# A kernel with a chunked linear recurrence: score matmuls per head over 64 rows, and the upper three levels' scores copied by ScalarE

## What is computed

```python
for t in range(S):
    cur = einsum('bhd,bhe->bhde', u * k[t], v[t])
    y[t] = einsum('bhd,bhde->bhe', r[t], state + cur)
    state = w[t][..., None] * state + einsum('bhd,bhe->bhde', k[t], v[t])
x = x + relu(norm(x) @ w_ch1) @ w_ch2
u_, v_ = split(relu(x @ w_in)); out = (u_ * (w_spatial @ norm(v_) + b)) @ w_out
```

## Time and profile before

| | |
|---|---|
| runs, median | 484.99 us (484.53 to 485.33) |
| profiled execution, span | 483.2 us, first to last instruction |
| TensorE busy | 438.5 us |
| VectorE busy | 282.0 us |
| ScalarE busy | 209.3 us |
| GpSimd busy | 150.2 us |

### The profile page before, as it was taken

The page is one execution under the profiler, slowest core; times in us unless marked ns, Lnnn a source line. Parts: engine busy times, 40 slices in busy tenths (PEclk is TensorE's granted clock), DMA queues, the critical chain, the costliest instruction groups (busy, mean ns, idle before and its releaser), DMA issues.

```text
span 483.2 us, 7994 instructions
## 1 busy us (share of the span) xinstructions
PE 438.5 (91%) x2724; PEld 413.5 (86%) x2724; DVE 282.0 (58%) x600; ACT 209.3 (43%) x486; POOL 150.2 (31%) x234
## 2 busy tenths in 40 slices
PE   3688779877877799999999999999999999999997
PEld 3587669776767689999999999999999998898997
DVE  6999999999999997124422432333241684413120
ACT  4787667667776673322212321332221752211211
POOL 6586666668776673600000000100010530000000
PEclk9999997799999999999999999999999999999999
DMA  7434432334432112200000000000410110010102
GB/s 222 139 79 118 116 99 72 85 92 123 124 85 72 50 36 68 65 1 0 1 0 1 1 1 1 0 1 0 152 44 1 33 34 2 0 50 1 50 1 97
DMA packets 26540, 25.59 MB, mean 53 GB/s; under 512 B 1666, under 2 KB 21890, under 8 KB 26500
## 3 DMA queue, kind: packets, MB, share of 16 engines
q1 hardware_dynamic: 26500, 25.08, 17.7%
HBM read 22.72 MB, written 2.36 MB: 52 GB/s over the span
## 4 chain that ended last, share of the span: by engine, by line
PE 63%; DVE 7%; issue 2%; ACT 1%; POOL 0%; DVEq 0%; ACTq 0%
PE bank L1122 20%; PE bank L1124 19%; PE bank L1123 19%; DVE score L773 3%; DVE wtot L731 2%; PE bank L1100 1%; PE bank L1207 1%; PE bank L1028 1%; DVE rin L750 1%; DVE sdec L804 1%; DVE ku L783 0%; PE bank L1069 0%; PE bank L1071 0%; PE bank L1070 0%; DVE state L820 0%
## 5 line engine op out<-in xcount | busy, mean ns | idle before, releaser
L1028 PE MATMUL bank<-rz,k 128*128 128x128 f32 x576 | 85.4, 295 | 28.9 <-DVE score L773 15.2
L1028 PEld LDWEIGHTS bank<-rz,k 128*128 128x128 f32 x576 | 74.3, 202 | 38.0 <-issue 36.7
L572 ACT COPY rz<-rin 64x256 f32<-64x256 f32 x144 | 58.7, 408 | 42.7 <-DVE rin L750 36.6
L773 DVE COPY_PREDICATED score<-msk,bank 128x512 f32<-128x512 int32 x84 | 74.0, 881 | 0.9
L511 POOL TENSOR_TENSOR vrstd<-vmv,half 128x1 f32<-128x1 f32 x12 | 7.7, 643 | 156.5 <-DVE vmv L974 156.5
L494 POOL TENSOR_TENSOR k<-k,wtot 128x256 f32<-128x256 f32 x60 | 42.8, 714 | 1.6
L466 POOL TENSOR_TENSOR k<-kin,ucol 128x128 f32<-128x128 f32 (+2 forms) x72 | 22.4, 311 | 54.5 <-ACT k L597 53.3
L887 DVE SCALAR_TENSOR_TENSOR h11l<-bank,h11h 128x384 fp32r<-128x384 f32 x24 | 13.4, 557 | 37.4 <-ACT h11h L660 37.4
L750 DVE TENSOR_TENSOR rin<-rin,wtot 128x256 f32<-128x256 f32 x60 | 32.8, 547 | 3.0 <-ACT rz L572 2.7
L660 ACT ACTIVATE h10h<-bank 128x384 fp32r<-128x384 f32 x24 | 11.8, 490 | 51.2 <-PE bank L1124 51.2
L887 DVE SCALAR_TENSOR_TENSOR h10l<-bank,h10h 128x384 fp32r<-128x384 f32 x24 | 13.4, 557 | 34.4 <-ACT h10h L660 34.4
(11 more groups left out here) (158 smaller groups left out, 1162.7 us busy)
## 6 DMA issues: line engine op xcount, KB each, us to landing
stage<-in_w SPq DMA_DIRECT2D x12, 384.0 KB, 3.3
vin<-in_v SPq DMA_DIRECT2D x12, 288.0 KB, 2.8
rin<-in_rT SPq DMA_DIRECT2D x12, 256.0 KB, 4.4
win<-in_wT SPq DMA_DIRECT2D x12, 256.0 KB, 3.6
kin<-in_kT SPq DMA_DIRECT2D x12, 256.0 KB, 4.4
out<-ob SPq DMA_DIRECT2D x12, 192.0 KB, 1.9
stage<-in_w_in SPq DMA_DIRECT2D x4, 384.0 KB, 3.2
x<-in_w_sp SPq DMA_DIRECT2D x4, 384.0 KB, 5.0
```

Source lines behind the costliest of these rows:

```text
L572: last = sc.copy(dst, src[lo:hi, :, :, :])
L773: ve.copy_predicated(dst, mb, src).then_inc(scores_placed, 1)
L1028: mm = te.matmul(b_level[n % 3][:, a * P:(a + 1) * P], kk[:, a, :], rz[l][:, a, :, :].rearrange("p e t -> p (e t)"), start=True, stop=True)
```

## The change

Two edits are made together. First, the padded `rz[l]` becomes `rc[l]`, the right half of r without padding, one copy of 128 partitions in place of two of 64. `level` issues eight matmuls where it issued four: each reads 64 partitions (one head) and 64 columns, the two heads of a pair write different banks of `b_level[n % 2]`, two pairs of banks in place of three banks. `b_y` has one bank in place of two. Second, levels 4, 5 and 6 (c = 16, 32, 64) are no longer selected by VectorE: ScalarE copies their whole blocks out of PSUM (`place_blocks`): 4, 2 and 1 copies. Since a block copy leaves the diagonal out, `with_u` runs for levels 0 to 3 alone, and the own term covers tokens 0, 16, 32 and so on (N_OWN = 8 of a tile) instead of token 0 alone, placed under a mask. The memsets of the padding go away.

```diff
@@ -309,6 +314,14 @@
             return sum(carries(j) and not first(j) for j in range(i + 1))
 
         HALF = [(0, 64), (64, 128)]
+
+        def level_taken(eng, n):
+
+            i, l = n // NL, n % NL
+            if l < N_MASKED:
+                eng.wait_ge(scores_placed, N_MASKED * i + l + 1)
+            else:
+                eng.wait_ge(blocks_placed, N_BLOCK * i + l - N_MASKED + 1)
 
         def split_waits(eng, n):
 
@@ -550,7 +562,7 @@
         def _(act):
             sc = nc.scalar
 
-            def pad(i, l):
+            def take_right(i, l):
 
                 q = i % 2
                 if l == 0:
@@ -561,18 +573,10 @@
                     src = halves(rin[i % 4][:, :, :], LEVELS[l])[1]
                 if i > 0:
                     act.wait_ge(level_done, NL * (i - 1) + l + 1)
-                elif l % 2 == 0:
-                    act.wait_ge(zeroed_by_pool, l // 2 + 1)
-                else:
-                    act.wait_ge(zeroed_by_vector, l // 2 + 1)
-                for e, (lo, hi) in enumerate(HALF):
-                    dst = rz[l][lo:hi, :, e, :]
-                    if l:
-                        dst = dst.rearrange("p a (m c) -> p a m c", c=LEVELS[l])
-                        last = sc.copy(dst, src[lo:hi, :, :, :])
-                    else:
-                        last = sc.copy(dst, src[lo:hi, :, :])
-                last.then_inc(padded_r_ready if l else padded_r0_ready, 1)
+                dst = rc[l][:, :, :]
+                if l:
+                    dst = dst.rearrange("p a (m c) -> p a m c", c=LEVELS[l])
+                sc.copy(dst, src).then_inc(right_r_ready if l else right_r0_ready, 1)
 
             def k_pairs(i):
 
@@ -616,6 +620,19 @@
                 if part != 0:
                     op.then_inc(weight_hi_ready, 1)
 
+            def place_blocks(i, l):
+
+                n, c = NL * i + l, LEVELS[l]
+                act.wait_ge(level_done, n + 1)
+                act.wait_ge(scores_placed, N_MASKED * (i + 1))
+                act.wait_ge(own_in_score, i + 1)
+                src = b_level[n % 2][:, :, 0:BANK // 2].rearrange("p e (a t) -> p e a t", a=NPR)
+                for m in range(P // (2 * c)):
+                    s0 = 2 * c * m
+                    last = sc.copy(score[i % 2][s0:s0 + c, :, :, s0 + c:s0 + 2 * c],
+                                   src[s0:s0 + c, :, :, m * c:(m + 1) * c])
+                last.then_inc(blocks_placed, 1)
+
             def take_kt(i):
                 act.wait_ge(k_turned, carried(i))
                 if i >= 2:
@@ -624,21 +641,21 @@
 
             def take_x(i):
                 act.wait_ge(y_done, i + 1)
-                sc.copy(x[:, i, :], b_y[i % 2][:, 0:D]).then_inc(x_ready, 1)
+                sc.copy(x[:, i, :], b_y[:, 0:D]).then_inc(x_ready, 1)
 
             def split_vn(i):
                 b, c = i // CH, i % CH
                 act.wait_ge(vn_ready, i + 1)
                 sc.copy(vns[b][0][:, c * DH:(c + 1) * DH], vn[:, i, :]).then_inc(vn_hi_ready, 1)
 
-            pad(0, 0)
+            take_right(0, 0)
             k_pairs(0)
             k_right(0, 0)
             for i in range(NT):
                 for l in range(1, NL):
-                    pad(i, l)
+                    take_right(i, l)
                     if l == 5 and i + 1 < NT:
-                        pad(i + 1, 0)
+                        take_right(i + 1, 0)
                     k_right(i, l)
                     if l == 2 and i >= 1 and carries(i - 1):
                         take_kt(i - 1)
@@ -754,22 +776,20 @@
 
                 q = i % 2
                 dve.wait_ge(level_done, NL * i + l + 1)
-                if NL * i + l > 0:
-                    dve.wait_ge(scores_placed, NL * i + l)
+                if i + l > 0:
+                    dve.wait_ge(scores_placed, N_MASKED * i + l)
                 if l == 0 and i >= 2:
                     dve.wait_ge(y_done, i - 1)
-                src = b_level[(NL * i + l) % 3][:, :].rearrange("p (h t) -> p h t", h=H)
-                mk = msk[:, l, :]
+                src = b_level[(NL * i + l) % 2][:, :, 0:BANK // 2].rearrange("p e (a t) -> p e a t", a=NPR)
+                heads = score[q][:, :, :, :].rearrange("p e a t -> p (e a) t")
+                mk = msk[:, l * P // 2:(l + 1) * P // 2]
                 if l == 0:
-                    dst = score[q][:, :, :].rearrange("p h (m two) -> p h m two", two=2)[:, :, :, 1]
+                    dst = heads.rearrange("p h (m two) -> p h m two", two=2)[:, :, :, 1]
                     mb = mk[:, None, :].to_broadcast([P, H, P // 2])
                 else:
                     c = LEVELS[l]
-                    dst = halves(score[q][:, :, :], c)[1]
-                    src = src.rearrange("p h (m c) -> p h m c", c=c)
+                    dst = halves(heads, c)[1]
                     mb = mk.rearrange("p (m c) -> p m c", c=c)[:, None, :, :].to_broadcast([P, H, P // (2 * c), c])
-                if l == NL - 1:
-                    dst, src, mb = dst[:, :, 0, :], src[:, :, 0, :], mb[:, :, 0, :]
                 ve.copy_predicated(dst, mb, src).then_inc(scores_placed, 1)
 
             def own_product(i):
@@ -780,21 +800,23 @@
                     dve.wait_ge(own_parts_set, 3)
                 if i >= 1:
                     dve.wait_ge(own_ruk_ready, 2 * i)
-                ve.tensor_tensor(ku0[:, :, :], kin[i % 3][:, :, 0:1], ucol[:, :, None], ALU.mult).then_inc(
-                    own_uk_ready, 1)
+                ve.tensor_tensor(ku0[:, :, :], kin[i % 3][:, :, 0:P:STEP], ucol[:, :, None].to_broadcast([P, NPR, N_OWN]),
+                                 ALU.mult).then_inc(own_uk_ready, 1)
                 dve.wait_ge(own_uk_ready, i + 1)
                 dve.wait_ge(r_in_sbuf[i % 2], 16 * (i // 2 + 1))
                 if i >= 2:
                     dve.wait_ge(own_summed, i - 1)
                 for e, (lo, hi) in enumerate(HALF):
-                    ve.tensor_tensor(ruk0[i % 2][lo:hi, :, e:e + 1], ku0[lo:hi, :, :], rin[i % 4][lo:hi, :, 0:1],
+                    ve.tensor_tensor(ruk0[i % 2][lo:hi, e, :, :], ku0[lo:hi, :, :], rin[i % 4][lo:hi, :, 0:P:STEP],
                                      ALU.mult).then_inc(own_ruk_ready, 1)
 
             def own_score(i):
                 dve.wait_ge(own_summed, i + 1)
                 if i >= 2:
                     dve.wait_ge(y_done, i - 1)
-                ve.tensor_copy(score[i % 2][0:1, :, 0], b_own).then_inc(own_in_score, 1)
+                at_own = msk[:, N_MASKED * P // 2:][:, None, :].to_broadcast([P, H, N_OWN])
+                ve.copy_predicated(score[i % 2][:, :, :, 0:P:STEP].rearrange("p e a j -> p (e a) j"), at_own,
+                                   b_own.rearrange("p (h j) -> p h j", h=H)).then_inc(own_in_score, 1)
 
             def decay_state(i):
 
...
@@ -927,14 +947,10 @@
                     if l == 0 and 3 <= i < 3 + TG:
                         norm(i - 3)
 
-                    if l >= 2:
+                    if 2 <= l < 2 + N_MASKED:
                         select(i, l - 2)
-                    elif i >= 1:
-                        select(i - 1, NL - 2 + l)
             decay_state(NT - 2)
-            select(NT - 1, NL - 2)
             next_state(NT - 2)
-            select(NT - 1, NL - 1)
             for n in range(EARLY):
                 h1_lo(n)
             for i in (NT - 2, NT - 1):
@@ -1013,8 +1029,8 @@
             def level(i, l):
 
                 n = NL * i + l
-                padded(te, i, l)
-                te.wait_ge(uk_ready, n + 1)
+                right_r(te, i, l)
+                te.wait_ge(uk_ready, N_MASKED * i + min(l + 1, N_MASKED))
                 if l == 0:
                     te.wait_ge(k_even_ready, i + 1)
                     kk = k1u
@@ -1022,11 +1038,12 @@
                     te.wait_ge(k_left_ready, NL * i + l)
                     te.wait_ge(k_right_ready, NL * i + l)
                     kk = kc[LEVELS[l]]
-                if n >= 3:
-                    te.wait_ge(scores_placed, n - 2)
+                if n >= 2:
+                    level_taken(te, n - 2)
                 for a in range(NPR):
-                    mm = te.matmul(b_level[n % 3][:, a * P:(a + 1) * P], kk[:, a, :],
-                                   rz[l][:, a, :, :].rearrange("p e t -> p (e t)"), start=True, stop=True)
+                    for e, (lo, hi) in enumerate(HALF):
+                        mm = te.matmul(b_level[n % 2][:, e, a * P // 2:(a + 1) * P // 2], kk[lo:hi, a, :],
+                                       rc[l][lo:hi, a, :], start=True, stop=True)
                 mm.then_inc(level_done, 1)
 
             def own_term(i):
@@ -1038,7 +1055,7 @@
                     te.wait_ge(own_in_score, i)
 
                     te.wait_ge(state_ready, 2 * carried(i - 2))
-                te.matmul(b_own, ones_c[:, :], ruk0[i % 2][:, :, :].rearrange("p a e -> p (a e)"),
+                te.matmul(b_own, ones_c[:, :], ruk0[i % 2][:, :, :, :].rearrange("p e a j -> p (e a j)"),
```

(13 more changed lines are left out.)

## The result

The changed kernel takes 569.18 us (568.86 to 569.68, four runs) against 485.0 us: a ratio of 1.174, interval 1.172 to 1.175. That is 84 us slower. The span went from 483.2 to 567.1 us.

A forecast was written before the change was run, and what follows sets the result against it. VectorE was taken to bound the attention stage. Tile ends -4.2, own terms +3.3, last tile +0.6 and clock +1.5 gave 486.2 us; 1.0 off for the memset made 485.2, own range 478 to 492, with rivals 471 to 502.

The forecast's parts named there:

- VectorE as the bound, and what leaves it: Attention stage: VectorE sets the pace; three selects, about 2.1 us a tile, leave it, net relief 1.8 us a tile.
- The own terms: VectorE's wider own-term work: 0.3 us more a tile, between 0.15 and 0.45, giving back 3.3 us over eleven tiles.
- ScalarE's chain: Tile end: ScalarE's block copies delay VectorE's next level 1 multiplication to 3.05 us after the level 3 select, from 2.40.
- The gap with a state: Level 3 select to next level 0 select, where a state is decayed: 7.6 us, from 8.0.
- A level on TensorE: Sixteen records of a level: 0.86 us if the two heads' loads and products overlap, 1.71 if loads go singly; overlap taken.
- Rival 2: TensorE becomes the bound: loads go one by one, a level takes 1.71 us, a tile 16.2; 501 us, chance 0.24.
- the switch between 64-row and 128-row matmuls: TensorE's tiling mode would switch some fourteen times a tile, each draining the engine; no price was known.
- The clock: TensorE's clock in the attention stage: one to three falls of 0.5 to 1 us each, 1.5 us in all.
- Rival 3: The clock falls in most tiles, about 1 us each in seven tiles instead of two: 490 us, chance 0.13.
- Rival 1: VectorE's relief is kept, block copies costing near 0.15 us each: 471 us, floor 463 after 22 us; chance 0.13.

The follow-up runs named there:

- The block copies alone: Changed kernel with padded r and four 128-row matmuls a level again, ScalarE's block copies kept: 488.26 us, ratio 1.0076.
- The unpaired order: Changed kernel with a level's four even-head matmuls first, then the four odd-head ones, so neighbours share their 64 rows: 633.74 us.
- the third experiment's second run: Changed kernel, each 64-row matmul streaming its 64 columns twice, 128 in all, the second half unused: 488.68 us.
- the dense start: Changed kernel with sixty bf16 matmuls of 128 x 256 on constants ahead of the first level, results unused: 569.13 us.
- the third experiment: Two variants of the changed kernel: level matmuls of 128 rows with 64 columns, 679.43 us; of 64 rows with 128 columns, 488.68 us.
- the last experiment: The block copies alone, with four level banks in place of two and the block copies moved behind the next tile's first copies: 475.77 us, ratio 0.9811.

## Why the prediction was wrong, step by step

**VectorE as the bound, and what leaves it.** Right. VectorE's selects went from 84 to 48. Its busy time over the kernel fell from 282.0 to 240.9 us, by 41 where I had some 20; twelve times the 2.1 us of selects is 26 us, and where the rest went was not followed up. The own terms cost more than I took: `own_score` 0.44 us in place of 0.15 us, so 0.29 more for that alone, where I had 0.15. The elements lie 64 bytes apart there and 8 in the select that I scaled from.

**ScalarE's chain.** Right in kind, and a little short. It shows only with the clock up: T + 3.70 against my 3.05 us, and VectorE waited 1.73 us there against my 1.9. The copies in a row did not overlap: four of level 4 took 1.06 us where I had 0.87, two of level 5 took 0.74 where I had 0.6. (By my own terms, 0.27 us each and 0.1 of overlap, four make 0.78, so the 0.87 does not follow from them.) The gap with a state is 7.7 against my 7.6, without one 6.4 to 6.8 against 5.8. The block copies alone ran 4.1 us over the kernel before (488.26 against 484.15), where the sum of all my terms was +0.2.

**A level on TensorE.** The overlap of the two heads, which I took for the likely case, is right: 1.04 us at full clock against my 0.86. Rival 2 had the bound right, TensorE, and the reason wrong: the loads do not go one by one. I had given it rows 7 and 8 as evidence that a load's price does not fall with the rows, but both are over 128 partitions and differ in columns alone. The unpaired order is the nearest thing to a test: 0.176 us a record over 64 rows against 0.21 over 128, at the low clock.

One term I left at nothing, the switch between 64-row and 128-row matmuls. In the third experiment's second run, at full clock, a pair of `attend` between two levels took 140.63 - 139.80 = 0.83 us in place of the 0.65 of the earlier trace rows, and `gain` 142.79 - 141.73 = 1.06 in place of 0.86. That is near 0.2 us for going over and back, with matmuls that were not changed. TensorE was not the bound there, so it cost little.

**The clock.** This is the step that failed. I wrote "I expect one to three falls and 0.5 to 1 us for each: 1.5 us", and gave the case of frequent falls 490 us. I reasoned from TensorE's idle time: the earlier trace rows show a fall behind a stretch in which it was busy for 1.51 of 3.41 us. For the falls this held: the eight of the block copies alone and that of the dense start came behind such waits. The wrong part was the other half, which I never wrote down: that a low stretch ends by itself once TensorE is busy. With 128 columns in a record it did, every time. In the changed kernel the clock was low while TensorE was busy for 176.67 of 178 us. The edit took columns out of each record, 64 behind a load of 128 where there had been 128, and the runs of the third experiment show that this went with the low clock, whatever the rows. In the change the clock, low at the start, did not come up in the whole attention stage, in the run with the dense start it fell at the first waits and stayed down, and at that clock the level's 1.90 us made TensorE the bound at 22.7 us a tile. I priced a fall as a delay that TensorE catches up, and a low clock without end was in none of my cases. What a level costs at that clock was in the trace of before: 1.98 us for its eight records at 71.96 us, against the 0.92 of the earlier trace rows.

**Rival 3**, a fall in most tiles, gave 490 us. The block copies alone are that case, with eight falls and 488.26 us. How much of its 4.1 us is the clock's and how much is ScalarE's chain was not told apart. In the changed kernel the clock did not fall often; it was never up.

**Rival 1**, the relief kept, came to 9 of its 22 us, but only in the last experiment, with the old matmuls and another order.

The Trainium skill, "TensorE: Matmul & The Clock Gate", says in its Part 1 that the lower level is the default and that activity lifts it. The runs agree in part: the dense start lifted it. The closing table of that page of the Trainium skill gives idle gaps between matmuls as what to avoid. The falls agree with that (busy for 1.20 of 3.41 us ahead of the one in the run with the dense start). But there were no gaps between 60 and 250 us of that run, and the clock was at 0.50 all the same, so gaps alone do not tell the level, and the measurement decides.

## What to carry to other kernels

Before cutting a matmul's columns to save TensorE's work, ask what is left behind each weight load: here the clock stayed at 1.2 GHz with 64 columns over the same rows, and was at 2.4 GHz nearly throughout with 128 columns, half of them wasted, 80 us apart. Ask of a fall in the clock not only what brings it on but what ends it. Read the clock from the spacing of a matmul that was not changed, not from busy time or from a clock column without a record. Where a slow engine's work goes to another one, look at what stands behind it in that engine's order: moving two copies went with 8 us (part of it the clock's), four banks and later copies with 12.

## What the runs showed of the hardware that I had not expected

- The clock stayed low for some 250 us with TensorE busy throughout, at 128 rows and 64 columns (679.4 us) as at 64 rows and 64 columns (569.2 us).
- More work made the kernel faster: four bf16 matmuls of 128 x 256 a level took it from 569.2 to 496.1 us, two made it 607.3 us.
- Waits came ahead of the clock's falls; what differed was the way back. With 128 columns in a record a low stretch ended with TensorE busy for 3.41 of 3.41 us, with 64 columns it outlasted 190 us of a busy TensorE.
- Two float32 matmuls over different 64 partitions and into different banks ran side by side: sixteen records with 128 columns in 1.10 us at full clock, against eight records over 128 partitions in 0.92. Going from 128-row matmuls to these and back cost near 0.2 us.
- What in the records' columns decides between the two levels was not tried further; there are runs at 64 and at 128 columns alone.
